# Attention, routing and feed-forward layers on one core: two experts' float32 products made from rounded matrices and their rests

## What is computed

```python
x = attention(q, k, v)                    # block/window attention -> 1536 rows of 512
# routing: 1536 tokens, 8 experts, each expert gets exactly cap = 192 tokens
for e in range(E):
    mask = assigned == e
    h = np.maximum(x[mask] @ w1[e], 0.0)  # 512 -> 1024
    out[mask] = h @ w2[e]                 # 1024 -> 512
# a dense layer over all 1536 rows
h = x @ w_in                              # 512 -> 1024, then softmax, gate, layer norm
return (ln @ w_out)                       # 1024 -> 512
```

## Time and profile before

| | us |
|---|---|
| median of three runs (491.86 to 494.44) | 492.03 |
| profiled execution, its own time | 497.49 |
| profiled execution, span from first to last instruction | 495.7 |
| PE busy | 475.7 (96%) |
| DVE busy | 344.3 (69%) |
| ACT busy | 159.1 (32%) |
| POOL busy | 137.4 (28%) |

### The profile page before, as it was taken

One profiled execution on the slowest core, in us unless ns is written; L12 is line 12 of the kernel. 1 busy time (PEld: TensorE's weight loads), 2 busy tenths in 40 slices (PEclk: granted clock), 3 DMA queues, 4 the chain that ended last, 5 costly groups with the idle time before them and its releaser, 6 DMA issues.

```text
span 495.7 us, 8454 instructions
## 1 busy us (share of the span) xinstructions
PE 475.7 (96%) x3022; PEld 416.5 (84%) x3022; DVE 344.3 (69%) x1094; ACT 159.1 (32%) x326; POOL 137.4 (28%) x213
## 2 busy tenths in 40 slices
PE   7999999999999999999999999999999999999992
PEld 4887788788789989779989988998998899899871
DVE  5577777779989898999869779987975610400451
ACT  3467778630021211433223123322302330220340
POOL 5466677840230220061131023113103241010101
PEclk9699999999999999999999999999999999999997
DMA  8966775110180450073352046034205528000001
GB/s 259 288 230 232 252 232 178 34 33 0 42 325 7 171 202 1 1 252 142 114 182 119 1 171 222 22 130 169 96 0 197 196 93 301 0 22 0 2 21 42
DMA packets 30040, 61.75 MB, mean 125 GB/s; under 512 B 6576, under 2 KB 19760, under 8 KB 25904
## 3 DMA queue, kind: packets, MB, share of 16 engines
q0 software_dynamic: 6592, 39.85, 22.0%
q1 hardware_dynamic: 22544, 20.53, 12.9%
q10 hardware_dynamic: 864, 0.84, 0.6%
HBM read 54.93 MB, written 6.29 MB: 123 GB/s over the span
## 4 chain that ended last, share of the span: by engine, by line
PE 84%; DVE 9%; DMA 2%; issue 2%; ACT 2%; POOL 0%; SPq 0%; DVEq 0%; ACTq 0%; POOLq 0%
PE psum L1128 17%; PE psum L1145 14%; PE psum L1210 5%; PE psum L917 5%; PE psum L1217 5%; PE psum L926 5%; PE psum L1211 4%; PE psum L1179 4%; PE psum L1180 4%; PE psum L1189 4%; PE psum L952 4%; DVE key_wide L1517 3%; PE psum L949 2%; PE psum L1157 2%; PE psum L1077 2%
## 5 line engine op out<-in xcount | busy, mean ns | idle before, releaser
L1517 DVE TENSOR_SCALAR_CACHE_REDUCE key_wide<-keys,thr 128x1536 bf16<-128x1536 f32 x49 | 88.7, 1810 | 1.1
L1145 PE MATMUL psum<-xs,w_sb 128*128 128x192 f32 x512 | 87.0, 328 | 0.0
L1128 PE MATMUL psum<-shared,w_sb 128*128 128x192 f32 x512 | 84.6, 326 | 0.2 <-ACT shared L810 0.2
L1128 PEld LDWEIGHTS psum<-shared,w_sb 128*128 128x128 f32 x512 | 83.4, 190 | 1.4 <-issue 0.9
L1145 PEld LDWEIGHTS psum<-xs,w_sb 128*128 128x128 f32 x512 | 83.0, 190 | 0.0
L680 POOL DMA_INDIRECT w_sb<-w,widx x32 | 31.4, 982 | 75.2 <-DVE widx L1597 66.8
L704 POOL TENSOR_TENSOR gain<-spread,cst 128x1 f32<-128x1 f32 x12 | 6.7, 562 | 163.3 <-DVE spread L1659 162.7
L1626 DVE TENSOR_TENSOR yT_lo<-psum,yT_hi 128x384 fp32r<-128x384 f32 x16 | 8.8, 553 | 51.7 <-ACT yT_hi L810 51.4
L1210 PE MATMUL psum<-wout_hi,turned_hi 128*128 128x512 f32 x96 | 38.6, 402 | 1.2 <-ACT turned_hi L810 1.2
L763 ACT ACTIVATE keys<-keys,nmax 128x184 f32<-128x184 f32 x96 | 37.4, 439 | 5.4 <-DVE nmax L1349 5.3
L1179 PE MATMUL psum<-win_hi,yT_hi 128*128 128x512 f32 x96 | 38.5, 402 | 0.0
(11 more groups left out here) (180 smaller groups left out, 816.1 us busy)
## 6 DMA issues: line engine op xcount, KB each, us to landing
shared<-vT SPq DMA_DIRECT2D x8, 384.0 KB, 6.5
shared<-v_main SPq DMA_DIRECT2D x8, 384.0 KB, 3.7
x_rows<-xs SPq DMA_DIRECT2D x8, 384.0 KB, 4.8
shared<-kT SPq DMA_DIRECT2D x7, 384.0 KB, 6.4
shared<-qT SPq DMA_DIRECT2D x7, 384.0 KB, 5.4
w_sb<-w_in SPq DMA_DIRECT2D x4, 512.0 KB, 5.3
w_sb<-w_out SPq DMA_DIRECT2D x8, 256.0 KB, 4.5
w_sb<-v_tail SPq DMA_DIRECT2D x16, 48.0 KB, 4.0
```

What stands on the lines that cost most here:

```text
L1128: mm = pe.matmul(turn[u % 2][:, i * CAP:(i + 1) * CAP], w1_sb[:, par, first:first + P], xT[:, c, :], start=(c == 0), stop=(c == KC - 1))
L1145: mm = pe.matmul(turn[u % 2][:, (d % 2) * CAP:(d % 2 + 1) * CAP], w2_sb[:, par, first:first + P], hT[:, c, :], start=(c == 0), stop=(c == ...
L1517: link(dve.tensor_scalar(hits, keys[:, :], cand, -float(CAP), ALU.is_ge, ALU.add, accum_out=count[:, :]))
```

## The change

For r = 6 both expert products, and for r = 7 the first one, are put into the split form. ACT rounds the gathered matrix in four pieces of 1024 columns into the other slot (`round_w1`, `round_w2`), and the rest is written over the original, two pieces by POOL (`split_w1`, `split_w2`) and two by DVE (`rest_of_w1`, `rest_of_w2`). Tokens and hidden values are kept as pairs [hi | lo], 384 columns. For each block of 128x128 weights there is one fp32r matmul of the rounded block with the whole pair, 384 columns, and one of the block's rest with the pair's hi half, 192 columns (`split_products`). They leave two partial sums side by side in a bank; DVE adds them (`add_pair`) into `pair_sum`, ACT takes Relu or copies from there, and DVE makes the rest (`split_hidden`, `split_pair_y`). A unit is now one block of output columns: `hidden` of these rounds has 8 units and y of r = 6 has 4. The rounded copies lie over buffers that are used up by then (`keys`, `key_wide`, `xs`, the other weight slot), so the gathers of round 7 wait for the products of round 6: that of w1 for its last `hidden` unit, that of w2 for its last y unit. For r = 6 POOL issues both weight gathers ahead of the tokens' gather. Two instructions of DVE at the program's very end are gone.

```diff
+SPLIT, SPLIT_Y = (E - 2, E - 1), E - 2
+PIECES, POOLED = 4, 2
...
+        h_high = rounded("h_high", [P, FC // 2, 2, CAP], next_address())
...
+        x_pair = rounded("x_pair", [P, KC, 2, CAP], next_address())
...
+        h_low = rounded("h_low", [P, FC // 2, 2, CAP], next_address())
...
+        w1_split = rounded("w1_split", [P, 2, KC * FF], next_address())
         w1_sb = sb("w1_sb", [P, 2, KC * FF])
+        w2_split = rounded("w2_split", [P, 2, FC * DM], next_address())
         w2_sb = sb("w2_sb", [P, 2, FC * DM])
+        pair_sum = sb("pair_sum", [P, 2, CAP])
...
-                gather_weights(r, w1, w1_sb, in_w1)
+                gather_weights(r, w1, w1_sb, in_w1, hidden_filled[r - 1] if r - 1 in SPLIT else y_filled[r - 2])
...
-                gather_weights(r, w2, w2_sb, in_w2)
+                gather_weights(r, w2, w2_sb, in_w2, y_filled[r - 1] if r - 1 == SPLIT_Y else y_filled[r - 2])
...
+            def split_w1(r):
+
+                k = SPLIT.index(r)
+                for j in range(POOLED):
+                    pool.wait_ge(w1_hi_ready, PIECES * k + j + 1)
+                    pool.tensor_tensor(w1_split[:, r % 2, piece(j)], w1_sb[:, r % 2, piece(j)],
+                                       w1_split[:, 1 - r % 2, piece(j)].bitcast(F32), ALU.subtract).then_inc(w1_lo_ready, 1)
...
-                if r + 1 < E:
+                if r + 1 == SPLIT_Y:
+                    gather_w1(r + 1)
+                    gather_w2(r + 1)
+                    gather_tokens(r + 1)
+                    split_w1(r + 1)
+                elif r == SPLIT_Y:
+                    gather_tokens(r + 1)
+                    gather_w1(r + 1)
+                    gather_w2(r + 1)
+                    split_w1(r + 1)
+                elif r + 1 < E:
...
+                if r + 1 == SPLIT_Y:
+                    split_w2(r + 1)
...
+            def empty_split_hidden(r, f):
+                k = SUMS * SPLIT.index(r) + f
+                act.wait_ge(sum_ready, k + 1)
+                act.activation(h_pair(f)[:, 0, :] if r == SPLIT_Y else hT[:, f, :], pair_sum[:, f % 2, :],
+                               ACT.Relu).then_inc(unit_emptied, 1)
+
+            def empty_split_y(r, d):
+                first = (r % 2) * CAP
+                act.wait_ge(sum_ready, FC + d + 1)
+                act.activation(yT_hi[:, d, first:first + CAP], pair_sum[:, d % 2, :], ACT.Copy).then_inc(unit_emptied, 1)
+
+            def round_w1(r, pieces):
+
+                act.wait_ge(in_w1[r % 2], 32 * (r // 2 + 1))
+                act.wait_ge(unit_filled, hidden_filled[r - 1])
+                for j in pieces:
+                    act.activation(w1_split[:, 1 - r % 2, piece(j)], w1_sb[:, r % 2, piece(j)],
+                                   ACT.Copy).then_inc(w1_hi_ready, 1)
...
+                if r == SPLIT_Y:
+                    round_w1(r + 1, range(PIECES))
...
+                        if first:
+                            round_w1(r + 1, range(2))
                         hidden_exp(n)
+                        if first:
+                            round_w1(r + 1, range(2, PIECES))
+                        if second:
+                            round_w2(r + 1, range(3, PIECES))
...
+                    if first:
+                        round_w2(r + 1, range(1))
...
+                    if first:
+                        round_w2(r + 1, range(1, 3))
...
-                if u >= 2:
+                if u - 2 in sum_unit:
+                    pe.wait_ge(sum_ready, sum_unit[u - 2])
+                elif u >= 2:
                     pe.wait_ge(unit_emptied, u - 1)
                 if u - 2 in y_unit:
                     pe.wait_ge(y_lo_ready, y_unit[u - 2])
+                if u - 2 in x_unit:
+                    pe.wait_ge(x_lo_ready, x_unit[u - 2])
...
+            def split_products(u, high, low, pair, first, last):
+
+                both = turn[u % 2][:, 0:2 * CAP]
+                if not last:
+                    pe.matmul(both, high, pair.rearrange("p s n -> p (s n)"), start=first, stop=False)
+                mm = pe.matmul(turn[u % 2][:, 0:CAP], low, pair[:, 0, :], start=False, stop=False)
+                if last:
+                    mm = pe.matmul(both, high, pair.rearrange("p s n -> p (s n)"), start=False, stop=True)
+                return mm
+
+            def hidden_split(r, f):
+
+                par, k = r % 2, SPLIT.index(r)
+                u = at["hidden", r] + f
+                if f == 0:
+                    pe.wait_ge(x_lo_ready, 2 * k + 2)
+                unit_free(u)
+                for c in range(KC):
+                    if f == 0 and c < POOLED:
+                        pe.wait_ge(w1_lo_ready, POOLED * k + c + 1)
+                    elif f == 0:
+                        pe.wait_ge(w1_rest_ready, (PIECES - POOLED) * k + c - POOLED + 1)
+                    cols = slice(c * FF + f * P, c * FF + (f + 1) * P)
+                    mm = split_products(u, w1_split[:, 1 - par, cols], w1_split[:, par, cols], x_pair[:, c, :, :],
+                                        c == 0, c == KC - 1)
+                mm.then_inc(unit_filled, 1)
...
+            def product_split(r, d):
+
+                par = r % 2
+                u = at["y", r, d]
+                unit_free(u)
+                for c in range(FC):
+                    if d == 0:
+                        pe.wait_ge(h_lo_ready, c + 1)
+                        if c % 2 == 0 and c // 2 < POOLED:
+                            pe.wait_ge(w2_lo_ready, c // 2 + 1)
+                        elif c % 2 == 0:
+                            pe.wait_ge(w2_rest_ready, c // 2 - POOLED + 1)
+                    cols = slice(c * DM + d * P, c * DM + (d + 1) * P)
+                    mm = split_products(u, w2_split[:, 1 - par, cols], w2_split[:, par, cols], h_pair(c), c == 0, c == FC - 1)
...
+            def add_pair(u, k):
+
+                dve.wait_ge(unit_filled, u + 1)
+                dve.tensor_reduce(pair_sum[:, k % 2, :], turn[u % 2][:, 0:2 * CAP].rearrange("p (s n) -> p n s", s=2),
+                                  AX.X, ALU.add).then_inc(sum_ready, 1)
+
+            def split_hidden(r, f):
+                dve.wait_ge(unit_emptied, at["hidden", r] + f + 1)
+                dve.scalar_tensor_tensor(h_pair(f)[:, 1, :], pair_sum[:, f % 2, :], 0.0, h_pair(f)[:, 0, :].bitcast(F32),
+                                         ALU.max, ALU.subtract).then_inc(h_lo_ready, 1)
...
+            def rest_of_w1(r):
+
+                for j in range(POOLED, PIECES):
+                    dve.wait_ge(w1_hi_ready, PIECES * SPLIT.index(r) + j + 1)
+                    dve.tensor_tensor(w1_split[:, r % 2, piece(j)], w1_sb[:, r % 2, piece(j)],
+                                      w1_split[:, 1 - r % 2, piece(j)].bitcast(F32), ALU.subtract).then_inc(w1_rest_ready, 1)
...
+            def split_expert(r):
+
+                for f in range(FC):
+                    if f >= 2:
+                        dve.wait_ge(h_lo_ready, f - 1)
+                    add_pair(at["hidden", r] + f, f)
+                    if f:
+                        split_hidden(r, f - 1)
+                split_hidden(r, FC - 1)
...
+            rest_of_w1(E - 2)
             hidden_max(m)
             split_turned(n)
             hidden_gate(m)
+            split_x(E - 2)
+            rest_of_w2(E - 2)
             hidden_spread(m)
-            for r in (E - 2, E - 1):
-                split_y(r, 0)
-                split_y(r, 1)
+            for r in SPLIT:
+                if r == SPLIT_Y:
+                    split_expert(r)
+                    rest_of_w1(r + 1)
+                else:
+                    last_hidden(r)
+                    split_y(r, 0)
+                    split_y(r, 1)
                 for n in tiles_after(r):
                     hidden_max(n)
                     split_turned(n - 1)
                     hidden_gate(n)
+                    if r + 1 < E:
+                        split_x(r + 1)
                     hidden_spread(n)
```

More of the change, by code:

```diff
@@ L143, in turns_keys, with hidden_units, y_units, y_before @@
     return r + 2 < ROUNDS and d == (1 if r % 2 == 0 and r else 3)
+def hidden_units(r):
+    return FC if r in SPLIT else FC // 2
+def y_units(r):
+    return KC if r == SPLIT_Y else KC // 2
+def y_before(r):
+    return sum(y_units(i) for i in range(r))
 def unit_order():
@@ L149, in unit_order @@
         yield ("tokens", r), 2
-        yield ("hidden", r), FC // 2
-        for d in range(KC // 2):
+        yield ("hidden", r), hidden_units(r)
+        for d in range(y_units(r)):
             yield ("y", r, d), 1
@@ L877, in _ @@
                     empty_tokens(1)
-                for n in tiles_after(r):
+                for i, n in enumerate(tiles_after(r)):
+                    first, second = ((r + 1, i) == (SPLIT_Y, k) for k in range(2))
                     if n >= 1:
@@ L1137, in product @@
                     pe.wait_ge(in_w2[par], 32 * (r // 2 + 1))
[L1138 removed]
+                    if r not in SPLIT:
```

(18 more changed lines are left out.)

151 lines of the change are left out of this document (113 added, 38 removed).

## The result

The changed kernel takes 498.21 us (median of 5 runs, 497.99 to 499.16), the kernel before 493.60 us on the same chip (5 runs, 491.86 to 494.44): a ratio of 1.0109, 95% interval 1.0090 to 1.0129. It is slower by 1.1%, about 5.4 us. The forecast was 489.0 us and faster; the time lies outside its range.

What follows compares the result with a forecast made beforehand. TensorE was taken to bound the kernel. Products -4.2, both `hidden` starts +0.9 and the end of y +0.25 summed to -3.05 us, from 492.03 to 489.0 us; range 485.8 to 493.8.

Steps and rivals of the forecast that it cites:

- What is hidden: Rounding and rests of rounds 6 and 7 fit into idle time of ACT, DVE and POOL, adding nothing to the path.
- Rival E: Expert products: short fp32r matmul no faster than its float32 record or a whole load; 493.1, 495.5 or 508.7 us; chance 0.18.
- The pair: Expert products: matmuls of 384 and 192 columns take 0.171 and 0.110, 0.281 us instead of 0.325; 4.2 us less over 96 blocks.
- what would show the prediction wrong: Expert products: the prediction is wrong if the spacing of the short matmuls is far from 0.110 us.
- B: Expert products: short matmul follows its columns, 0.083, long one 0.1625, together 0.2455 us; 486.2 us in all; chance 0.12.
- The start of `hidden`: Rounds 6 and 7: TensorE waits for DVE's first sum to free a bank, 0.45 us each, 0.9 for both.
- The end of y: Round 6: dense tile 9 waits for `yT_hi`, since a sum now precedes ACT's copy; 0.25 us.
- DVE's sum: Split products: sum 0.55 and subtraction of 192 columns 0.36, 0.91 us per unit against PE's 1.125; DVE keeps up.
- C: Split products: DVE's sum takes 0.95, so DVE needs 1.31 us a unit against 1.125; 491.3 us in all; chance 0.15.
- Round 7's w1: Gather and ACT's rounding finish before `empty_turned(8)` at 424.7, covered by 0.6 us; no cost.
- D: Round 7: w1's gather or ACT's four pieces overrun the 0.6 us; at 2 us over, 490.4 us; chance 0.08.
- ACT's roundings: Round 6: eight activations of 1024 columns, 1.06 us each at most, stand in ACT's gaps; uncovered they would cost 8.4 us.

Runs made afterwards that it cites:

- version 7: Changed kernel with one wait added: POOL's two w1 pieces of round 6 begin after DVE's last one-hot; 1.0033 of the kernel before, 494.32 us.
- version 2: Changed kernel with all w1 rests of rounds 6 and 7 made by DVE, none by POOL; 1.0014 of the kernel before, 493.59 us.
- version 1: Changed kernel with all four w1 rests of round 6 made by DVE, round 7 unchanged; 1.0066 of the kernel before, 496.22 us.
- 3 to 6: Four runs of the kernel before with added POOL work (subtractions, copies, memsets, subtractions without a wait between): 1.0071, 1.0073, 1.0064, 1.0081 of the kernel before.
- version 8: version 2 with one DVE rest of round 6 moved ahead of `hidden_spread(7)` and POOL's w2 pieces waiting for DVE's four w1 rests; 0.9992, 492.07 us.
- version 9: version 8 with POOL's two w2 pieces moved ahead of `gain(7)` and its scatter; 0.9955 of the kernel before, 489.68 us beside 492.46.
- version 3: Kernel before with the changed kernel's gather order and two POOL subtractions of 1024 columns on dead memory, a wait between them; 1.0071 of the kernel before.
- version 5: Kernel before with the changed kernel's gather order and five POOL memsets of 1024 columns, which only write; 1.0064 of the kernel before.
- version 6: Kernel before with two POOL subtractions of 768 columns on separate dead data, no wait between them; 1.0081 of the kernel before.

## Why the prediction was wrong

The step that failed is the one under "What is hidden": "POOL's four take 2.36 each; two need 4.7 us, and POOL idled 4.63 us before 390.25", and beside it DVE's four "1.22 each", with "DVE's two pieces end at 425.3" for round 7 (they ended at 429.66). Each engine's work was laid into its own idle time, and the two lists were never laid beside each other. The durations were right where nothing collided (POOL 4.73 us for two; DVE 2.35 for two in version 7, and 4.66 for four in round 7 of version 2). But of two instructions that want the same ports one waits, and `slotv`, 0.17 us long, stands between TensorE and its work. The prediction put at nothing, without a reason, that DVE and POOL wait for each other; no term and no rival had it, nor the lower clock behind the pause (2.37 us of it). The loss, 6.34 + 2.72 = 9.1 us, is three times the gain I forecast. Rival E had a slower kernel, but by the products, and only to 495.5. The cause was shown from three sides: with the w1 rests taken from POOL both losses go (1, 2), POOL work given to the kernel before brings the first (3 to 6), and moving POOL's pieces in time takes the first away (7).

The other steps, by their own numbers:

- *The pair.* 0.281 was forecast for 0.325. A stage of 32 pairs takes 9.15 us (y(6): 410.34 to 419.49), 0.286 a pair, against 10.33 before: 1.19 us for each of three products, 3.6 in all instead of 4.2. By their starts the long matmul takes some 0.19 and the short one 0.09, where I had 0.171 and 0.110. The long one is above my upper bound for it (0.174), the short one below the 0.110 by which I named what would show the prediction wrong; that the two errors cancel but for 0.005 is luck. B and E fall: the pair is neither 0.2455 nor over 0.32. The Trainium skill's load rule (TensorE: Matmul & The Clock Gate, LDWEIGHTS) had given an estimate of 0.278; the measured pair is a little above it.
- *The start of `hidden`,* 0.45 us each. In round 6: 18.74 us for two stages of 9.15, so 0.44. In round 7 of the changed kernel nothing shows, since `hidden(7)` was late itself; where it isn't (2, 8, 9) the last column is 0.36 to 0.38 longer. The mechanism held.
- *The end of y,* 0.25: measured 0.34 (6.87 instead of 6.53).
- *DVE's sum* takes 557 ns, the rest of 192 columns 351: DVE keeps up with a unit's 1.14 us, and C falls.
- *Round 7's w1:* its gather was issued at 411.31, the rounding ran from 420.77 to 424.67, and `empty_turned(8)` at 425.62 had 0.95 us of idle time ahead of it: covered, by slightly more than the 0.6 forecast. D falls. ACT's roundings cost nothing, as forecast.

Summed: -3.6 + 0.44 + 0.37 + 0.34 = -2.4 us. That is what version 9 shows, which has the same products with the rests laid otherwise: -2.33 us by its profile and -2.2 by its ratio. The forecast of -3.05 was thus right to some 0.7 to 0.9 us for everything but the ports, and wrong in sign with them.

One reading of the rows was wrong and changed nothing: the earlier trace rows has the clock under 0.90 in the second slice (0.6) and the last, not in the first.

## What to carry to other kernels

Before work is laid into idle time of POOL, lay DVE's timeline beside it and mark DVE instructions with two SBUF inputs, and those from SBUF to SBUF with one; DVE work with an input in PSUM is a safe cover (beside POOL's w2 pieces in version 9 `hneg`, `turned_lo` and the product behind them took 1.21, 1.27 for two and 1.22 us, as before), and POOL's own small instructions have to be kept from DVE's long ones in the same way. Look for the shortest such instruction that TensorE waits for: it is the one that pays. A late start of TensorE can cost more than its own length, by the lower clock behind it: 3.97 us cost 6.34 here.

## What the runs showed of the hardware

- A DVE addition of 12 columns with both inputs in SBUF took 4.20 us beside two POOL subtractions issued back to back (2.37 us beside two of 1.45), and ended with the second. Where POOL waited for a semaphore between its instructions, it ended with the first (1.37 us, version 3).
- POOL doesn't always keep the ports for its next instruction: a DVE subtraction of 1024 columns with two SBUF inputs (version 1, 3.43 us) and a `TENSOR_SCALAR` of 1024 columns (version 7, 1.23 us) got in between two POOL pieces, whose second then took 3.35 and 2.85 us instead of 2.39. What decides is open.
- A DVE addition with two SBUF inputs was not held by POOL memsets (0.17 us, version 5); the twelve `TENSOR_SCALAR` with one SBUF input were (4.85 us instead of 2.33).
- The other way: POOL's `gain` of one column took 0.56 us alone and 3.75 beside three DVE subtractions in a row (version 8), and ended after the third; beside two in a row (changed kernel, 388.21 to 390.56) it took 1.48 and was done before the second.
- The granted clock was 0.50 for about 7 us (0.89, 0.50 three times and 0.90 in five stretches of 2 us) behind 1.85 us idle and 2.88 us of 24 matmuls of two columns, and for a shorter time behind 0.73 us and 2.62 us (version 3). It stayed at 1.00 with the same 2.62 us and no idle time before it in the profiled execution of version 6, and behind 1.38 us idle followed by eight matmuls of 128 columns and then full ones (changed kernel, from 431.65).
- The same stretch of program can lose clock in one execution and not in another: 0.64, 0.50 and 0.84 from 10 to 25 us in the profile of the kernel before, 1.00 in that of version 3, whose program differs only from round 5 on.
